# Attention front in whole 32-bit floats: scores and P·V of the first 16 steps without splits, normalising on GpSimd

## The reference

```python
scores = scale * np.matmul(q, k.transpose(0, 1, 3, 2))
thresh = np.max(scores, axis=-1, keepdims=True) - tau
scores = np.where(scores >= thresh, scores, -1000000000.0)
scores = scores - np.max(scores, axis=-1, keepdims=True)
attn = np.exp(scores)
attn = attn / (np.sum(attn, axis=-1, keepdims=True) + 1e-09)
x = np.matmul(attn, v)                     # then to (tokens, 512)
h = x @ w_in;   x = (h * (1.0 / (1.0 + np.exp(-1.702 * h)))) @ w_out
h = x @ w_in2;  y = (h * np.tanh(np.log1p(np.exp(h)))) @ w_out2
```

## Time and profile before

| what | us |
|---|---|
| median of 3 runs | 1164.22 (1163.97 to 1164.56) |
| the profiled execution | 1164.77 |
| its span in the profile | 1163.0 |
| PE busy in the span | 1102.5 (95%) |
| DVE, ACT, POOL busy | 774.3, 738.7, 315.8 |

### The profile page before, as it was taken

One profiled execution on the slowest core, in us unless ns is written; L12 is line 12 of the kernel. 1 busy time (PEld: TensorE's weight loads), 2 busy tenths in 40 slices (PEclk: granted clock), 3 DMA queues, 4 the chain that ended last, 5 costly groups with the idle time before them and its releaser, 6 DMA issues.

```text
span 1163.0 us, 19459 instructions
## 1 busy us (share of the span) xinstructions
PE 1102.5 (95%) x7472; PEld 1037.8 (89%) x7472; DVE 774.3 (67%) x1383; ACT 738.7 (64%) x1019; POOL 315.8 (27%) x526
## 2 busy tenths in 40 slices
PE   6678889999999999999999999999999999999998
PEld 5568889998999999999999999998999989899997
DVE  6978788888888888888888533665433444344343
ACT  6878787867777777778767322467545554554453
POOL 6876674434444433344333000000000000000000
...
DMA packets 93948, 80.43 MB, mean 69 GB/s; under 512 B 47520, under 2 KB 79264, under 8 KB 93856
## 3 DMA queue, kind: packets, MB, share of 16 engines
...
## 4 chain that ended last, share of the span: by engine, by line
PE 74%; DVE 13%; ACT 7%; issue 4%; POOL 0%; DMA 0%; ACTq 0%; DVEq 0%
PE ps_s L693 17%; PE ps_r L577 13%; PE ps_r L598 11%; PE ps_r L716 9%; PE ps_t L449 5%; PE ps_t L463 5%; PE ps_t L716 4%; PE ps_s L436 4%; PE ps_t L598 3%; DVE pt_lo L519 2%; DVE neg_max L499 2%; DVE x_pair L533 2%; ACT pv_half_sb L495 2%; DVE e_buf L506 2%; DVE q_st L400 2%
## 5 line engine op out<-in xcount | busy, mean ns | idle before, releaser
L577 PE MATMUL ps_r<-x_hi,wi_lo 128*128 128x256 f32 x544 | 158.7, 292 | 1.9 <-DVE x_lo L651 1.9
L760 DVE COPY hidden<-ps_s 128x768 f32<-128x768 f32 x48 | 45.8, 956 | 170.5 <-PE ps_s L693 170.5
L449 PE MATMUL ps_t<-ident,e_buf 128*128 128x128 f32 x720 | 118.8, 285 | 38.6 <-DVE pt_lo L519 27.5
L577 PE MATMUL ps_r<-x_lo,wi_hi 128*128 128x256 f32 x544 | 154.4, 284 | 0.0
L577 PE MATMUL ps_r<-x_hi,wi_hi 128*128 128x256 f32 x544 | 154.4, 284 | 0.0
L487 ACT CAST pt_hi<-ps_t 128x640 fp32r<-128x640 f32 x144 | 100.1, 695 | 82.7 <-PE ps_t L449 80.2
L789 ACT ACTIVATE m_lo_raw<-m_lo_raw 128x1536 f32<-128x1536 f32 x24 | 35.8, 1491 | 168.8 <-DVE m_lo_raw L767 168.8
L449 PEld LDWEIGHTS ps_t<-ident,e_buf 128*128 128x128 f32 x720 | 85.9, 144 | 58.9 <-issue 29.6
L598 PE MATMUL ps_r<-g_hi,wo_lo 128*128 128x256 f32 x464 | 135.3, 292 | 0.0
L693 PE MATMUL ps_s<-x_hi,wi_lo 128*128 128x384 f32 x384 | 129.0, 336 | 2.4 <-DVE x_lo L749 2.4
L598 PE MATMUL ps_r<-g_lo,wo_hi 128*128 128x256 f32 x464 | 130.9, 282 | 0.0
...
## 6 DMA issues: line engine op xcount, KB each, us to landing
...
```

Of the source, the lines that this page charges most:

```text
L449: mm = pe.transpose(t_flat[:, j * P:(j + 1) * P], e_buf[n % 3][:, j * P:(j + 1) * P], ident[:, :])
L577: mm = pe.matmul(bank[:, part * CH:(part + 1) * CH], wi[w][:, k, f * P:(f + 1) * P], x[:, k, :], start=t == 0, stop=t == 3 * KT - 1)
```

## The change

For the front steps alone the splits go. The query rows are scaled in place (`act_q_scale`), the scores are two products of whole 32-bit floats per step on 64 rows of the array, P·V is five such products per head with 64 output rows, and one ACT copy (`act_x_first`) takes the result. The casts and subtractions of queries, keys, values and weights (P) of these steps are gone; the copy of the transposed tile stays, now without a cast. All 16 steps are normalised on POOL. The loads of keys and queries for these steps take 64 partitions instead of 128; those of the queries wait for a later event than before (the scores of the last step on that buffer instead of their split). From step 16 on nothing is computed in another way.

```diff
@@ -260,9 +259,9 @@
             kind, h, i, u, _ = STEPS[n]
-            if n < FRONT and (n // 2) % 2 == 1:
+            if n < FRONT:
                 cols = slice((n % 2) * P, (n % 2 + 1) * P)
-                return pt2_hi[:, :, cols], pt2_lo[:, :, cols]
+                return ((pt_raw, pt2_raw)[(n // 2) % 2][:, :, cols],)
             if kind == "tails":
@@ -376,12 +383,19 @@
+
+        def act_q_scale(act, u):
+            lo, hi = q_span(USES[u][2])
+            q = q_raw[u % 2][0:D, lo:hi]
+            act.wait_ge(q_in[u % 2], 16 * (u // 2 + 1))
+            act.activation(q, q, ACT.Copy, scale=SCALE).then_inc(s["q_scaled"], 1)
+
         def act_k_hi(act, u):
...
         def pool_k_lo(pool, u):
-            pool.wait_ge(s["k_hi"], u + 1)
+            pool.wait_ge(s["k_hi"], u - H + 1)
             for half in range(2):
@@ -408,28 +422,41 @@
             v = v_st[u % 2]
-            pool.wait_ge(s["v_hi"], u + 1)
+            pool.wait_ge(s["v_hi"], u - H + 1)
             pool.tensor_tensor(v[:, :, D:P], v_raw[u % 2][:, :, D:P], v[:, :, 0:D].bitcast(F32),
...
-        KQ_PREP, Q_LO, V_PREP = ({}, {}, {})
+        Q_SCALE, KQ_PREP, Q_LO, V_PREP = ({}, {}, {}, {})
         for u, first in enumerate(FIRST):
+            if u < H:
+                Q_SCALE.setdefault(max(first - 3, -1), []).append(u)
+                continue
             for table, at_ in ((KQ_PREP, first - 3), (Q_LO, first - 2), (V_PREP, first + 2)):
-                table.setdefault(max(at_, -1), []).append(u)
+                table.setdefault(at_, []).append(u)
...
             if FIRST[u1] == n:
-                pe.wait_ge(s["q_lo"], u1 + 1)
+                if u1 < H:
+                    pe.wait_ge(k_in[u1 % 2], 16 * (u1 // 2 + 1))
+                    pe.wait_ge(s["q_scaled"], u1 + 1)
+                else:
+                    pe.wait_ge(s["q_lo"], u1 - H + 1)
             if n >= 2:
                 pe.wait_ge(s["masked"], n - 1)
+            if n < FRONT:
+                for half in range(2):
+                    mm = pe.matmul(scores(n)[:, half, :], q_raw[u0 % 2][0:D, q_cols(h, i)],
+                                   k_raw[u0 % 2][0:D, half * HS:(half + 1) * HS], start=True, stop=True)
+                mm.then_inc(s["qk_done"], 1)
+                return
             terms = [(h, u0)] if kind == "full" else [(h, u0), (h + 1, u1)]
...
                 if FIRST[u1] == n:
-                    pe.wait_ge(s["k_lo"], 2 * u1 + half + 1)
+                    pe.wait_ge(s["k_lo"], 2 * (u1 - H) + half + 1)
                 cols = slice(half * HS, (half + 1) * HS)
@@ -440,11 +467,13 @@
                 if normed_by_pool(n):
-                    pe.wait_ge(s["normed_even"], n // 2 + 1)
+                    pe.wait_ge(s["normed_first"], n + 1)
                 else:
-                    pe.wait_ge(s["normed"], (n + 1) // 2 if n < FRONT else n - FRONT // 2 + 1)
-                if n >= 1:
-                    pe.wait_ge(s["p_lo"], n)
+                    pe.wait_ge(s["normed"], n - FRONT + 1)
+                if 1 <= n <= FRONT:
+                    pe.wait_ge(s["p_hi"], n)
+                elif n > FRONT:
+                    pe.wait_ge(s["p_lo"], n - FRONT)
             for j in tiles:
@@ -452,16 +481,23 @@
             _, _, _, u, last = GROUPS[g]
-            pe.wait_ge(s["p_lo"], last + 1)
-            pe.wait_ge(s["v_lo"], u + 1)
-            if g >= 2:
-                pe.wait_ge(s["pv_sum"], g - 1 if g < H else g)
-            hi, lo = pv_moving(g)
             w = group_cols(g)[1]
+            if g < H:
+                pe.wait_ge(s["p_hi"], last + 1)
+                pe.wait_ge(v_in[u % 2], 16 * (u // 2 + 1))
+                if g >= 2:
+                    wait_sums(pe, g - 1)
+                v, out_rows = v_raw[u % 2][:, :, D:P], slice(0, D)
+            else:
+                pe.wait_ge(s["p_lo"], last + 1 - FRONT)
+                pe.wait_ge(s["v_lo"], u - H + 1)
+                wait_sums(pe, g)
+                v, out_rows = v_st[u % 2], slice(0, P)
+            parts = pv_moving(g)
             for j in range(NJ):
-                for part, pt in enumerate((lo, hi)):
-                    mm = pe.matmul(pv_bank(g)[:, 0:w], v_st[u % 2][:, j, :], pt[:, j, :],
-                                   start=j == 0 and part == 0, stop=j == NJ - 1 and part == 1)
+                for part, pt in enumerate(parts):
+                    mm = pe.matmul(pv_bank(g)[out_rows, 0:w], v[:, j, :], pt[:, j, :],
+                                   start=j == 0 and part == 0, stop=j == NJ - 1 and part == len(parts) - 1)
             mm.then_inc(s["pv_done"], 1)
@@ -473,7 +509,7 @@
-            return n < FRONT and n % 2 == 0
+            return n < FRONT
@@ -490,9 +526,14 @@
             act.wait_ge(s["pv_done"], g + 1)
-            if g >= 1:
-                act.wait_ge(s["pv_sum"], g)
+            wait_sums(act, g)
             act.copy(pv_half_sb[base:base + D, 0:w], pv_bank(g)[D:P, 0:w]).then_inc(s["pv_half"], 1)
+
+        def act_x_first(act, g):
+            h = GROUPS[g][1]
+            base = (h % 2) * D
+            act.wait_ge(s["pv_done"], g + 1)
+            act.copy(x_raw[base:base + D, h // 2, 0:256], pv_bank(g)[0:D, 0:256]).then_inc(s["x_first"], 1)
@@ -672,7 +710,7 @@
         X_HI = {slot - 2: c for c, slot in START_SLOT.items() if c >= 1}
-        X_HI_FIRST = {max(GROUPS[2 * k + 1][4] + 4, 0) if k < KT - 1 else GROUPS[2 * k + 1][4] + 3: k for k in range(KT)}
+        X_HI_FIRST = {GROUPS[2 * k + 1][4] + 3: k for k in range(KT)}
@@ -895,12 +933,12 @@
                     act_tanh(act, pair)
-                turn_first = n < FRONT + 2 or n - 3 not in GROUP_AT
+                turn_first = n < FRONT + 3 or n - 3 not in GROUP_AT
                 if turn_first and 0 <= n - 2 < N:
...
                     act_g_hi(act, pair)
-                if n >= FRONT + 2 and n - 3 in GROUP_AT:
+                if n >= FRONT + 3 and n - 3 in GROUP_AT:
                     act_pv(act, GROUP_AT[n - 3])
@@ -908,8 +946,10 @@
                     act_exp(act, n)
-                if n < FRONT + 2 and n - 4 in GROUP_AT:
-                    act_pv(act, GROUP_AT[n - 4])
+                if n < FRONT + 3 and n - 3 in GROUP_AT:
+                    act_x_first(act, GROUP_AT[n - 3])
+                for u in Q_SCALE.get(n, []):
+                    act_q_scale(act, u)
                 for u in KQ_PREP.get(n, []):
@@ -973,10 +1013,8 @@
                     dve_x_lo_first(dve, X_HI_FIRST[n - 1])
-                if 0 <= n - 2 < N:
+                if FRONT <= n - 2 < N:
                     dve_p_lo(dve, n - 2)
-                if n < FRONT + 2 and n - 4 in GROUP_AT:
-                    dve_pv(dve, GROUP_AT[n - 4])
                 for pair in ups_at(n - 2):
@@ -1036,16 +1074,20 @@
             b, h, _ = USES[u]
+            rows = slice(0, D if u < H else P)
             if u >= 2:
                 sp.wait_ge(s["qk_done"], LAST[u - 2] + 1)
-            sp.dma_start(k_raw[u % 2], kt[b, h]).then_inc(k_in[u % 2], 16)
+            sp.dma_start(k_raw[u % 2][rows, :], kt[b, h][rows, :]).then_inc(k_in[u % 2], 16)
...
             b, h, cols = USES[u]
+            rows = slice(0, D if u < H else P)
             lo, hi = q_span(cols)
-            if u >= 2:
-                sp.wait_ge(s["q_lo"], u - 1)
-            sp.dma_start(q_raw[u % 2][:, lo:hi], qt[b, h, :, lo:hi]).then_inc(q_in[u % 2], 16)
+            if 2 <= u < H + 2:
+                sp.wait_ge(s["qk_done"], LAST[u - 2] + 1)
+            elif u >= H + 2:
+                sp.wait_ge(s["q_lo"], u - H - 1)
+            sp.dma_start(q_raw[u % 2][rows, lo:hi], qt[b, h, rows, lo:hi]).then_inc(q_in[u % 2], 16)
@@ -1071,7 +1113,7 @@
                         sp_k(sp, u)
-                    if max(FIRST[u] - 5, 0) == n:
+                    if (LAST[u - 2] - 1 if u < H + 2 else FIRST[u] - 5) == n:
                         sp_q(sp, u)
```

More of the change, by code:

```diff
@@ L195, in thresholded_attention_two_mlps @@
         wi, wo = [wi_hi, wi_lo], [wo_hi, wo_lo]
-        pt_hi, pt_lo = cut("att", "pt_hi", NJ, 384), cut("att", "pt_lo", NJ, 384)
+        (pt_hi, pt_raw), pt_lo = cut_both("att", "pt_hi", NJ, 384), cut("att", "pt_lo", NJ, 384)
         q_raw = [cut("att", f"q_raw{n}", SP_, dt=F32) for n in range(2)]
@@ L238, in thresholded_attention_two_mlps @@
         names = ("tau_in x_in y_out x2_in zeroed ident_ready ready "
-                 "q_hi k_hi v_hi q_lo k_lo v_lo w_hi w_lo w_lo_too w2_lo "
-                 "qk_done maxed thr_ready share_ready exped masked eps_ready inverted normed_even normed turned "
-                 "p_hi p_lo pv_done pv_half pv_sum "
+                 "q_scaled q_hi k_hi v_hi q_lo k_lo v_lo w_hi w_lo w_lo_too w2_lo "
+                 "qk_done maxed thr_ready share_ready exped masked eps_ready inverted normed_first normed turned "
+                 "p_hi p_lo pv_done x_first pv_half pv_sum "
                  "x_hi_done x_lo_done up_done tanh_done h_read g_hi_done g_lo_done down_done y_read "
@@ L278, in pv_moving @@
```

(42 more changed lines are left out.)

8 lines of the change are left out of this document (4 added, 4 removed).

## The result

The changed kernel took 1171.75 us (median, 1171.33 to 1172.75) against 1164.39 (1163.97 to 1164.65) in the same comparison: a ratio of 1.006, 95% interval 1.0047 to 1.0074 (every ratio below is to the kernel before, run beside it). It is 0.6% slower; the forecast was 1162.7, faster. The profiled execution took 1171.65, its span is 1169.9 us, 6.9 above that of before.

What follows compares the result with a forecast made beforehand. DVE, ACT and POOL, not PE, were taken to bound the front. Slot 14's transposes: 20.7 + 5 x 6.55 + 2.55 = 56.0 against 58.14; first MLP product 1.5 us earlier, so 1162.7 us by the median; range 1156.5 to 1174.

Steps and rivals of the forecast that it cites:

- the full clock by about 12 us: Start of the kernel: PE, nearly unbroken from 4.5 us, would have granted clock near 1 from about 12 us on.
- the first transposes behind P·V at 20.7: End of the start, slot 4: transposes behind the first P·V at 20.7 us against 21.93, 1.2 us won.
- Rival B: Front rounds: the low clock stays and PE binds, rounds about 10 us, 21 us more in six, 1184 us; chance 0.13.
- The sign that I named: Start, as evidence of a right forecast: granted clock near 1 from about 12 us on.
- Slot 8, priced at 1.9 us: Slot 8: POOL's norm and threshold wait behind ACT's P·V copy and weight cast, so the mask loses 1.9 us.
- From slot 14 on: Slot 14's transposes at 56.0 us to first MLP product at about 75.75; slot 14 loses 1.9 us.
- four runs per product: Front scores and P·V: each whole-float product takes four runs, 0.55 us for 288 columns, 0.48 for 256.
- A: Front products: whole floats cost little more than transposes, 1155.5 us; chance 0.15 together with an exact 2.4 GHz rate (1160.3).
- C: Front products: weight loads show, 0.12 us each, giving 1167.7 us if once per product, 1183 us if more often; chance 0.14.
- D: First MLP stage: it takes the gain, waiting for ACT's and DVE's unmoved preparations, 1164.2 us; chance 0.10.
- the loop of 6.55 us: Front rounds: transposes, copy, exp, mask, scores and P·V in sequence take 6.55 us a round against 7.24.
- The 0.65 us for small delays: Slots 6 and 10 (first-token split behind the copy) and 11 and 12 (POOL late): 0.65 us lost together.

Runs made afterwards that it cites:

- 128 rows alone: Changed kernel with front score products over 128 array rows instead of 64, queries and keys loaded doubled, scale halved: 1166.5 us, ratio 1.0008.
- both edits: Changed kernel with front scores over 128 rows and first MLP weight casts in slots 9, 11, 13, 16 instead of 8, 11, 14, 16: 1160.16 us, ratio 0.9964.
- the pair of 64 and 128 rows: Changed kernel with front loads and scaling over 128 partitions, score products on 64 rows (1172.8 us) or on 128 with halved scale (1166.5 us).

## Why the prediction was wrong

The forecast put the first MLP product at 75.75; it came at 83.99, 8.24 later. By its own terms:

- **What failed: the full clock by about 12 us, and with it the first transposes behind P·V at 20.7.** They came at 25.44: 4.74 of the 8.24. I took the level from PE being unbroken and priced the start at the full rate. Where the full rate is there the sum holds: 21.09 with 128 rows alone and 20.73 with both edits. Two things speak against what I took. The trace of before, which I could have read, was itself at the lower level through its first P·V (rows below): products of scores 0.24 us apart and of P·V 0.21, where the full rate gives 0.137 and 0.119. Doubling such work costs nearly twice what it costs at the full rate. And PE unbroken on 64-row products does not raise the level: 7.50 of 7.50 us busy, still 2.21 a step. Rival B named the half-empty array but put it at 0.13 and for whole rounds; at the start it acts only until the first P·V or just behind it. The sign that I named, a granted clock near 1 from 12 us on, could not tell: it read 1.00 at 2.21 us a step. The Trainium skill says in "TensorE: Matmul & The Clock Gate", section "What's actually happening", that the clock follows how busy the engine has been lately. By that alone I would have 9.2 to 21.8 at 2.4 GHz; the trace disagrees, and the pair of 64 and 128 rows shows that busy time by this profile is not all that counts.
  PE's timeline of the kernel before, scores of its start and the end of its first P·V:

```profile
19.08 0.44 PE L436 MATMUL ps_s<-k_hh,q_st 128*128 128x288 f32 x1
19.32 0.44 PE L436 MATMUL ps_s<-k_ll,q_st 128*128 128x288 f32 x1
...
21.50 0.41 PE L463 MATMUL ps_r<-pt_lo,v_st 128*128 128x256 f32 x1
21.72 0.41 PE L463 MATMUL ps_r<-pt_hi,v_st 128*128 128x256 f32 x1
```

- **Slot 8, priced at 1.9 us.** The chain was right and cost 2.18; the P·V at the low level behind the stall (1.69) was not in the sum. The round is 10.39 for a forecast 8.45, 1.94 more.
- **From slot 14 on** 22.09 us for 19.75, 2.34 more; P·V at the low level (4.34 for 2.37) is 1.97 of that.
- **Right: four runs per product.** At full rate 1.16 to 1.17 us a step and 2.30 from P·V to the transposes, against 1.19 and 2.38. The Trainium skill's four passes ("FP8 and Floating Point Precision", section "TensorE Precision Notes") give the same sum; the trace agrees. So rivals A and C fall. D falls by the version with both edits: from 53.63 to the first MLP product it takes 18.54 us against 19.11 before, so the stage behind passes the gain on.
- **Right: the loop of 6.55 us;** 6.52 measured, by its own terms: 2.17 from the transposes to the mask (2.12 in the sum), 0.89 to the scores (0.86), 1.16 and 2.30 for scores and P·V (1.19 and 2.38). The 0.65 us for small delays did not come (-0.78 over four rounds). A round without a stall, in the changed kernel:

```profile
31.96 0.76 PE L478 MATMUL ps_t<-ident,e_buf 128*128 128x128 f32 x5
...
32.77 0.69 ACT L523 COPY pt_hi_raw<-ps_t 128x640 f32<-128x640 f32 x1
33.36 0.74 ACT L507 ACTIVATE e_buf<-ps_s,neg_max 128x576 f32<-128x576 f32 x1
34.13 0.82 DVE L547 SCALAR_TENSOR_TENSOR e_buf<-ps_s,neg_thr,e_buf 128x576 f32<-128x576 f32 x1 [0.81 <-ACT e_buf L507]
35.02 1.24 PE L452 MATMUL ps_s<-k_ll_raw,q_raw 64*128 64x288 f32 x4 [0.43 <-DVE e_buf L547]
36.18 2.37 PE L499 MATMUL ps_r<-pt_hi_raw,v_st_raw 128*64 128x256 f32 x10
```

Together 4.74 + 1.94 + 2.34 - 0.78 = 8.24. Without the low level at the start and with the casts moved, the kernel runs at 1160.16: the round was forecast correctly, and the gain it gives, 3.6 us in five rounds against rounds of 7.24, is there. It went to 3.5 us at the start, 3.9 in slot 8 and 3.0 behind slot 14 (22.09 for 19.11): -3.6 + 3.5 + 3.9 + 3.0 = 6.8, the 6.74 seen.

Open: which property of the 64-row products holds the level down (rows loaded, or operand traffic), as only 64 and 128 rows were run; whether P·V, with 64 columns in use, raises it by itself; and why some stalls are followed by the low level and others not. Not run either was the kernel before with its weight casts in the odd slots, so how much of the 1160.16 is due to the whole floats and how much to the new slots is not shown.
